# The 128-point transform with its table's high and low halves in one matmul, its sums in a buffer, and its third tile a slot later

## The reference, cut to what matters

```
X = np.fft.fft(x, axis=1)          # over the 4224 tokens
X = np.fft.fft(X, axis=2)          # over the 192 channels
mixed = np.real(X)
u = x + mixed
un = (u - mean(u)) / sqrt(var(u) + 1e-6)
out = u + relu(un @ w_ch1) @ w_ch2
```

## Time and profile before

| what | value |
|---|---|
| time, median of 3 runs (lowest, highest) | 1247.24 us (1245.2, 1247.64) |
| the profiled execution: its own time, its span | 1249.38 us, 1247.6 us |
| granted TensorE clock, mean share of full speed | 0.993 |
| TensorE busy | 1217.3 us (98%) |
| VectorE busy | 829.9 us (67%) |
| ScalarE busy | 678.7 us (54%) |
| GpSimd busy | 424.3 us (34%) |
| DMA | 154.48 MB, mean 124 GB/s |

### The profile page before, as it was taken

One profiled execution on the slowest core, in us unless ns is written; L12 is line 12 of the kernel. 1 busy time (PEld: TensorE's weight loads), 2 busy tenths in 40 slices (PEclk: granted clock), 3 DMA queues, 4 the chain that ended last, 5 costly groups with the idle time before them and its releaser, 6 DMA issues.

```text
span 1247.6 us, 23842 instructions
## 1 busy us (share of the span) xinstructions
PE 1217.3 (98%) x8404; PEld 1189.8 (95%) x8404; DVE 829.9 (67%) x2238; ACT 678.7 (54%) x1779; POOL 424.3 (34%) x541
## 2 busy tenths in 40 slices
PE   6899999999999999999999999999999999999998
PEld 5799999999998999999999999999999999999998
DVE  5565576777675577655556877765666777766564
ACT  5355555444566655445555666544445656655554
POOL 0133342343343245323333344521212344433331
PEclk9899999999999999999999999999999999999999
DMA  9867543344556533224434322322333233232221
GB/s 293 277 210 222 177 142 91 106 135 135 162 182 215 183 115 97 75 69 133 130 105 136 118 88 90 94 63 76 92 101 107 71 110 96 90 99 86 75 74 35
DMA packets 87967, 154.48 MB, mean 124 GB/s; under 512 B 11480, under 2 KB 47043, under 8 KB 87804
## 3 DMA queue, kind: packets, MB, share of 16 engines
q1 hardware_dynamic: 80232, 133.95, 34.0%
q0 software_dynamic: 7616, 18.99, 4.8%
HBM read 94.59 MB, written 63.32 MB: 127 GB/s over the span
## 4 chain that ended last, share of the span: by engine, by line
PE 93%; DMA 2%; DVE 2%; POOL 1%; SPq 1%; issue 1%; ACT 1%; ACTq 0%; POOLq 0%
PE bank L811 20%; PE bank L812 9%; PE bank L792 8%; PE bank L799 7%; PE bank L800 7%; PE bank L796 7%; PE bank L793 7%; PE bank L815 4%; PE bank L910 3%; PE bank L845 2%; PE bank L873 2%; PE bank L933 2%; PE bank L875 2%; PE bank L874 2%; PE bank L814 2%; PE bank L894 2%
## 5 line engine op out<-in xcount | busy, mean ns | idle before, releaser
L1005 ACT ACTIVATE ht<-bank 128x384 fp32r<-128x384 f32 x528 | 259.0, 491 | 472.0 <-PE bank L800 470.7
L1201 DVE SCALAR_TENSOR_TENSOR ht<-bank,ht 128x384 fp32r<-128x384 f32 x528 | 293.7, 557 | 332.7 <-ACT ht L1005 329.0
L811 PE MATMUL bank<-w,ht 128*128 128x384 f32 x1320 | 418.6, 366 | 0.8 <-DVE ub L1209 0.5
L812 PE MATMUL bank<-w,ht 128*128 128x192 f32 x1320 | 330.9, 251 | 0.0
L1460 POOL TENSOR_TENSOR ub<-ub,tmp 128x576 f32<-128x576 f32 x87 | 124.4, 1430 | 452.2 <-DVE ub L1209 310.6
L811 PEld LDWEIGHTS bank<-w,ht 128*128 128x128 f32 x1320 | 248.9, 189 | 3.9 <-issue 3.1
L812 PEld LDWEIGHTS bank<-w,ht 128*128 128x128 f32 x1320 | 252.4, 191 | 0.0
L792 PE MATMUL bank<-uth,w1h 128*128 128x384 f32 x528 | 189.4, 359 | 0.0
L799 PE MATMUL bank<-uts,w1s 128*128 128x384 f32 x528 | 179.0, 339 | 0.6 <-DVE uts L1234 0.6
L796 PE MATMUL bank<-utl,w1h 128*128 128x384 f32 x528 | 178.9, 339 | 0.5 <-DVE utl L1226 0.5
L793 PE MATMUL bank<-uth,w1l 128*128 128x384 f32 x528 | 178.8, 339 | 0.0
(11 more groups left out here) (127 smaller groups left out, 2273.4 us busy)
## 6 DMA issues: line engine op xcount, KB each, us to landing
f1t<-f_copy SPq DMA_DIRECT2D x44, 396.0 KB, 3.3
ub<-x_two SPq DMA_DIRECT2D x44, 288.0 KB, 3.1
mix<-mixed SPq DMA_DIRECT2D x44, 288.0 KB, 3.3
out<-ub SPq DMA_DIRECT2D x43, 288.0 KB, 2.1
xin<-in_x SPq DMA_DIRECT2D x12, 864.0 KB, 7.1
x_conv<-xin SPq DMA_DIRECT2D x12, 756.0 KB
vch<-v_split SPq DMA_DIRECT2D x42, 192.0 KB, 2.8
mixed<-rowk SPq DMA_DIRECT2D x88, 74.2 KB
```

What stands on the lines that cost most here:

```text
L811: e.matmul(dn[t][:, 0:2 * D], hh, w2[ph][:, m, :], start=(m == 0), stop=False)
L812: mm = e.matmul(dn[t][:, 0:D], hl, w2[ph][:, m, 0:D], start=False, stop=False)
L1005: e.activation(hth[q % 4], up[q % 3][:, 0:TOK], ACT.Relu).then_inc(act_h, 1)
L1201: e.scalar_tensor_tensor(htl[q % 4], up[q % 3][:, 0:TOK], 0.0, hth[q % 4].bitcast(F32), ALU.max, ALU.subtract).then_inc(dve_l, 1)
```

## The change

Every transform is cut in its three tiles. A tile's six matmuls become five: for the first 128 channels the high part of the data is multiplied with the table's high and low half side by side (264 columns, one load of the weights), and the low part with the high half (132 columns); the last 64 channels keep three matmuls of 132 columns, in the same bank at columns 264 to 395. The product with the low half therefore stands in other columns than the rest, and must be added: ScalarE copies the main sum to a buffer `zt`, VectorE adds the other columns to it (`tile_sum`). Tiles 0 and 1 stand in the transform's slot (banks 0 and 1), tile 2 in a later slot, usually the next one (bank 0). When all three sums are there, ScalarE rounds `zt` into `zh` (`spectrum_high`), and VectorE takes the low part in the slot after that. The put-off transforms are six, not seven; what is stored and fetched is the folded `xf` (288 KB once), and rounding and rest are made after the fetch. The last transform of batches 1 to 3 moves from (n1, 4) to (n1, 3), that of batch 0 from (11, 5) to (11, 4), the last but one of batch 0 from (11, 3) to (11, 1). The convolution of batch 2 takes other slots, and its partial sum `t` uses bank 1. The table's request stands in the third tile's slot.

The diff, cut to its core:

```diff
-PUT_OFF = 7
+PUT_OFF = 6
...
+        zt = sb("zt", [128, TB * 2 * KC], F32)
...
         for b in range(B):
+            n0, n1 = at[(0, b, 0)], at[(0, b, 0)] + NB
             for u in range(NB):
                 w = b * NB + u
+                fold_at[w] = (n0 + u // 2 * 2 + 2, 1 if u % 2 == 0 else 3) if u < NB - 1 else (n1, 1)
                 if w in later:
+                    put_at[slot_after(*fold_at[w], 2)] = w
+                    spot = (n1 + 1 + u // 2, u % 2 * 3)
+                    made, third = slot_after(*spot, -1 if u % 2 == 0 else -2), slot_after(*spot, 1)
+                elif u < NB - 2:
+                    made, spot, third = [(n0 + u + 2, m) for m in (2, 4, 5)]
+                elif u == NB - 2:
+                    made, spot, third = (n1 - 1, 5), (n1, 0 if b else 1), (n1, 1 if b else 3)
+                else:
+                    made, spot, third = [(n1, m) for m in ((1, 3, 4) if b else (3, 4, 5))]
+                made_at[made], dft_at[spot], third_at[third] = w, w, w
+                split = slot_after(*third, 2) if w not in later and u < NB - 3 else third
+                split_at[split], split_low_at[slot_after(*split, 1)] = w, w
...
-            def dft128(n):
+            def dft_tile(w, t):
+                k = dft_order.index(w)
+                if t == 0:
+                    e.wait_ge(f1_in[k % 2], (k // 2 + 1) * 16)
+                    e.wait_ge(dve_x2l, k + 1)
+                bk, q = empty(e, ("dft", w, t))
+                xh, xl, wave, both = x2h[:, t], x2l[:, t], f1t[:, k % 2, 0, t, :], f1t[:, k % 2, :, t, :]
+                e.matmul(bk[:, 0:4 * KC].rearrange("p (a c) -> p a c", a=2), xh[:, 0:128], both, start=True, stop=False,
+                         skip_group_check=True)
+                e.matmul(bk[:, 0:2 * KC], xl[:, 0:128], wave, start=False, stop=True, skip_group_check=True)
+                o = bk[0:64, 4 * KC:6 * KC]
+                e.matmul(o, xh[:, 128:D], wave, start=True, stop=False, skip_group_check=True)
+                e.matmul(o, xh[:, 128:D], both[:, 1], start=False, stop=False, skip_group_check=True)
+                e.matmul(o, xl[:, 128:D], wave, start=False, stop=True, skip_group_check=True).then_inc(pe_tb[q], 1)
...
-            def spectrum_high(n):
+            def tile_out(w, t):
+                if t == 0:
+                    wait(e, dve_zl, dft_order.index(w))
+                o, q = full(e, ("dft", w, t))
+                copy(zt[:, t * 2 * KC:(t + 1) * 2 * KC], o[:, 0:2 * KC])
+                copy(spectrum_row(zs[0:64], w, t), spectrum_part(o[0:64], 2)).then_inc(act_tb[q], 1)
+            def spectrum_high(w):
+                k = dft_order.index(w)
+                e.wait_ge(dve_zt, (k + 1) * TB)
+                for rows, part in zip(spectrum_rows(zh[:], w), spectrum_sums(w)):
+                    last = copy(rows, part)
+                last.then_inc(act_zh, 1)
...
+            def spectrum_low(w):
+                e.wait_ge(act_zh, dft_order.index(w) + 1)
+                for low, part, high in zip(spectrum_rows(zl[:], w), spectrum_sums(w), spectrum_rows(zh[:], w)):
+                    last = e.tensor_tensor(low, part, high.bitcast(F32), ALU.subtract)
+                last.then_inc(dve_zl, 1)
+            def tile_sum(w, t):
+                o, q = copied(e, ("dft", w, t))
+                row = zt[:, t * 2 * KC:(t + 1) * 2 * KC]
+                e.tensor_tensor(row, o[:, 2 * KC:4 * KC], row, ALU.add).then_inc(dve_zt, 1)
+                e.tensor_tensor(spectrum_row(zs[64:128], w, t), spectrum_part(o[0:64], 2),
+                                spectrum_row(zs[0:64], w, t).bitcast(F32), ALU.subtract).then_inc(tb_free[q], 1)
...
                     if m + 2 < M6:
                         lows(n, m + 2)
...
+                    if (n, m) in split_low_at:
+                        spectrum_low(split_low_at[(n, m)])
+                    if (n, m) in third_at:
+                        tile_sum(third_at[(n, m)], 2)
...
                     if (n, m) in dft_at:
-                        spectrum_low(dft_at[(n, m)])
+                        for t in range(2):
+                            tile_sum(dft_at[(n, m)], t)
+                    if (n, m) in made_at:
+                        x2_low(made_at[(n, m)])
```

More of the change, by code:

```diff
@@ L332, in program @@
-        fetch_at = {((n - 1, 5) if m == 0 else (n, 1)): w for (n, m), w in dft_at.items() if w in later}
+        assert dft_order == [third_at[spot] for spot in sorted(third_at)] == [made_at[spot] for spot in sorted(made_at)]
+        made_of = {w: spot for spot, w in made_at.items()}
+        xf_before = {}
+        for half in range(2):
+            held = [(spot, w, "folded") for w, spot in fold_at.items() if w % NB % 2 == half]
+            for w in later[half::2]:
+                ahead_ = max((made_of[v], v) for v in fold_at if v % NB % 2 == half and made_of[v] < made_of[w])
+                fetch_at[slot_after(*ahead_[0], 1)] = w
+                held.append((slot_after(*ahead_[0], 1), w, "fetched"))
+            held.sort()
+            for k in range(1, len(held)):
+                xf_before[held[k][1:]] = held[k - 1][1:]
@@ L422, in program @@
         f1_in = [sem(f"f1_in{n}") for n in range(2)]
+        x2_out = [sem(f"x2_out{n}") for n in range(2)]
+        x2_in = [sem(f"x2_in{n}") for n in range(2)]
         u_in = [sem(f"u_in{n}") for n in range(UR)]
@@ L1176, in _ @@
                         turned_high(nx)
+                    if (n, m) in split_at:
+                        spectrum_high(split_at[(n, m)])
                     if (n, m) in dft_at:
-                        spectrum_high(dft_at[(n, m)])
+                        for t in range(2):
+                            tile_out(dft_at[(n, m)], t)
                     if (n, m) in made_at:
@@ L1235, in turned_low @@
                                     ALU.subtract).then_inc(tb_free[q], 1)
-            def xf_free(w):
-                before = max([v for v in range(w) if v % NB % 2 == w % NB % 2], default=-1)
-                wait(e, act_x2h, before + 1)
-                wait(e, dve_x2l, before + 1)
             def fold_sum(n):
```

154 lines of the change are left out of this document (67 added, 87 removed).

## The result

The change makes the kernel slower: 1280.07 us (median of 4 runs, 1277.61 to 1284.35) against 1247.44 for the kernel before (1245.2 to 1248.04), a ratio of 1.0272 [1.0258, 1.0286]. I had predicted 1242.1 in a range of 1229 to 1252. The profiled execution has a span of 1275.7 us; before it was 1247.6.

What follows compares the result with a forecast made beforehand. TensorE, busy in 98% of the span, was taken as the bound. 9.2 us gained, 6.0 lost and 2.0 gained made 5.2 us less than the median of 1247.24, so 1242.1 us, in a range of 1229 to 1252.

Steps and rivals of the forecast that it cites:

- usual transforms: Transforms in slots 4 and 5, 30 of 44: nothing waits, 0.31 us gained each, 9.2 us in all.
- the last two of each batch: Last two transforms of a batch: batches 1 to 3 lose 2.0 us each, 6.0 in all; batch 0 comes to 0.
- the put-off ones: Six transforms in blocks 23 to 25: 1.8 us saved by merging, 5.0 by old waits, 4.8 lost, net 2.0 gained.
- the merge on TensorE: The 264-column matmul takes 0.122 us, a tile 0.420, a transform gets 0.31 us shorter, 44 of them 13.5 us.
- Rival D: A matmul costs its columns alone, so the merge on TensorE saves nothing: 1255.5 us, chance 0.03.
- C: Rival: in the usual blocks the low-rank product waits 0.2 us for its bank, 30 times: 1248.1 us, chance 0.12.
- the fetch wait: TensorE's wait of 1.78 us for a fetch at a put-off transform goes, as half the bytes are asked for earlier.
- the waits at the last transforms: Blocks 22, 44 and 66: TensorE waits 2.0 us at the last transform's first tile, until VectorE's `turned_low` ends.
- the tails at 2.0 each: Ends of batches 1 to 3: 0.6 us for `utl` plus a 2.0 wait, less 0.6 from merging, 2.0 lost each.
- Batch 0's last two: Batch 0's last two transforms save 0.6 us and spend it on bank waits: 0.
- the 0.587 for the low part of the sums: VectorE's instruction of 396 columns in each transform was assumed to take 0.587 us.
- rival B: The clock falls in new waits at tails and put-off blocks, 1.7 us each: 1247.2 to 1252.3 us, chance 0.18.

Runs made afterwards that it cites:

- experiment 1: The changed kernel with the merge undone, the 264-column matmul being two of 132 columns again: 1289.92 us, ratio 1.0354.
- experiment 2: The changed kernel with `spectrum_low` of slot 2 moved behind `turned_low` and `x2_low` on VectorE: 1266.22 us, ratio 1.0161.
- experiment 5: The kernel before with 24 merged transforms, the product into `t` on bank 1, and GpSimd's `second_low` moved to blocks 13, 15 and 17: 1246.34 us, ratio 0.9996.
- experiment 15: The version of experiment 5 with the product into `t` ahead of the third tile, banks exchanged, where a slot has both: 1245.7 us, ratio 0.9994.
- experiment 13: The changed kernel with `x2_high` ahead of `spectrum_high` on ScalarE where both stand in the third tile's slot: 1276.78 us, ratio 1.0228.
- experiments 7 and 8: Two edits of the changed kernel, each alone. 7: two `zt` buffers, 1275.42 us. 8: `spectrum_low` of slot 0 ahead of `add_residual`, 1277.02 us.
- experiment 10: The changed kernel with `spectrum_low` cut to one of its 66 columns in batches 1 to 3: 1263.4 us, ratio 1.0133.
- the last versions: Experiment 15 with block 24's put-off transform in slot 1 and its product into `t` in slot 0, with 24 or 27 merged transforms: 1242.57 and 1243.13 us.

## Why the prediction was wrong

The sum forecast 5.2 us less; 32.6 more were measured, 28.1 in the profiled executions. With the convolution's moved work set at its price, the rows of the table give, forecast against measured: usual transforms (the 23 in blocks 3 to 10, 36 to 43 and 58 to 64) -7.1 against +1.2; the last two of each batch +6.0 against 19.3 (4.0 + 3.4 + 5.3 + 6.6); the put-off ones with blocks 26 and 27 -2.0 against +5.4; blocks 20 and 21, for which there was no term beyond two usual transforms, +2.6. These are estimates, from 1.7 for a step, 1.5 for a product and the tiles' own times.

**Right: the merge on TensorE.** 0.122 for the wide matmul and 0.31 a transform; measured 0.12 and 0.25 in blocks 58 to 64, where the split over two slots takes 0.05 back (experiment 1). Rival D is out. Right too: the low-rank product waits for no bank (not C), the fetch wait is gone, and the waits at the last transforms are ended by `turned_low` (1.66 and 1.68 in blocks 44 and 66, 0.40 in block 22; 2.0 forecast for each).

**Wrong: the usual transform "with nothing waiting".** I placed `spectrum_low` ahead of `turned_low`, checked only the up-projection behind it, and priced the rest at nothing. TensorE waits 0.31 to 0.35 us for `x2_low` in each of four blocks in a row (94.79 to 140.47, and again from 603.55 on), and experiment 2 removes just these. It is not the queue: `x2_low` starts as before (124.30 against 124.28 in block 5). `spectrum_low` holds up GpSimd, and GpSimd then holds up `x2_low` (1.32 instead of 0.90). The term that failed is the low part from SBUF, taken as if no other engine stood beside it. Blocks 5, 7, 38 and 40 had a second, smaller loss: in the version of experiment 5 the product into `t` cost 0.3 there until it went ahead of the third tile (experiment 15). Only the blocks without a convolution, 58 to 64, and the first of a row (3 and 36) kept their share of the 9.2 us.

**Wrong: the tails at 2.0 each.** Measured 4.0 to 6.6, since the sum followed one instruction to one wait. Three more were there to be found in the diff. The new wait of `spectrum_high` for the third sum stands ahead of `x2_high`: I wrote that the queue behind it "is part of the delay below" and gave it no number; it was 1.33, of which the order of the two is 0.8 (experiment 13). The one buffer `zt` ties ScalarE's next transform to VectorE's last low part: 1.24 (experiments 7 and 8). The mixing waits for the last low part: 0.7 and 1.1. Batch 0's last two, put at 0, cost 2.3 with a step of the convolution less beside them, some 4.0 without that.

**Wrong: the 0.587 for the low part of the sums.** I took it from a row whose first operand was in a bank. With both operands in SBUF it is 0.60 alone and 1.57 or 1.58, four times, beside GpSimd's addition. The Trainium skill ("SBUF — State Buffer", section "Who interferes with whom") has this rule: a VectorE instruction with two SBUF inputs contends with a GpSimd instruction that reads SBUF, the shared access is an exclusive lock, and the order of issue decides who is blocked. By experiment 10, the trace agrees: six columns took 1.15 instead of 0.16. Block 5 shows the other order, GpSimd held by VectorE. It is the rule against this change, and I had not weighed it.

**Too small: the put-off transforms.** 1.6 for each of three blocks; the main wait alone is 1.77 to 1.94, and in two of three the clock fell behind it, as rival B had it. Net +1.0 instead of -2.0, and that with one step of the convolution (eight matmuls, 1.7 us) and one product into `t` (1.5) moved out of these blocks.

**Left out: the convolution's new slots.** Seven of the eight places of its steps in batch 1 are new, some next to transposes and transforms; I gave the move no term. In blocks 20 and 21 TensorE waits 0.87 (`utl`), 1.30 (`zs`) and 0.88 (`utl`), 3.05 together.

So rival B had the sign and part of the mechanism, but its price came only from falls of the clock; in the profiled execution two more falls than before are some 3.2 of 28.1 us, the rest plain waits. The chances were added up wrongly too: by their own words "the same" is 0.06 + 0.09 + 0.08 = 0.23 and "slower" 0.13, not 0.18 each.

What stays open is the split between the queue's order and GpSimd's interference, and between the causes in the tails: the experiments overlap (13.9 alone in experiment 2, 4.7 in 7, 3.1 in 8, the last two not clear of noise, and 15.4 for the three). No run takes GpSimd's work for the convolution away and leaves the order, and the convolution's new slots were not undone by themselves.

## What to carry to other kernels

On an engine that runs its list in order, follow each inserted instruction not to the next reader but through everything queued behind it until the first pause, and do so for the engine that waits on it too. Then ask which instruction of the neighbouring engine runs at that moment, in both directions: here 0.6 us of work at the head of a slot cost 14 us over the kernel, in part as a delay in its own queue and in part through GpSimd, and moving it behind the rest of the slot gave them back. Before work moves from PSUM into a buffer in SBUF, see what GpSimd does at that time, and count the buffers. A shorter path on the bound engine pays only where its helpers have room: all 44 transforms merged lost 2.7%, 24 merged ones came out even (0.9994), and the 0.35% that the last versions are under the kernel before are mostly a fetch that got covered.

## What the runs showed that I had not expected

- A VectorE instruction with both inputs in SBUF that starts behind a GpSimd instruction is held until about that one's end: 128 x 396 took 0.60 alone, 1.58 beside an addition of 1.43 and 2.24 beside a subtraction of 2.39, and ended 0.45 us after it both times. In the other order GpSimd is held: its pair of 2.24 took 2.66 behind a `spectrum_low` that began 0.02 before it. The low part with its first input in a bank took 0.60 beside GpSimd's work as well (416.67 in the kernel before).
- The same wide matmul takes 0.12 us behind one of 384 columns (931.88) and 0.17 behind four of 132 (932.25), and 132 columns with 128-wide weights take 0.06 when they stand behind the wide one, where such matmuls in a row had 0.112. So in these rows what a matmul takes from start to start hangs on its neighbours' columns.
- ScalarE's copy of 64 x 132 into every 33rd element takes 0.405 us, 128 x 132 into neighbouring ones 0.294.
- A wait of TensorE is not always followed by a fall of the clock: behind 1.92 and 1.77 it fell, behind 1.94 it did not (granted clock 1.00), and behind the same 1.62 in block 32 it fell in some profiled executions (18.0 us) and not in others (16.4).
